# Multiplying a 64-row weight tail as two half-array products

## The reference

```
w    = softmax(weight, axis=-1)                 # 8 heads, 7 taps
conv[s, head] = sum_k w[head, k] * x[s + k - 6, head]      # causal, along the sequence
h1   = conv @ w_in1      (192 x 2048);  g1 = h1 * cos(h1);               y1 = g1 @ w_out1
h2   = y1 @ w_in2        (192 x 2048);  g2 = h2 * clip(h2 + 3, 0, 6)/6;  out = g2 @ w_out2
```

## Time and profile before

| | us |
|---|---|
| median of 3 runs | 2409.83 (2409.76 to 2409.97) |
| the profiled execution | 2408.54 |
| its span, first to last instruction | 2406.8 |
| TensorE matmul busy | 2367.1 (98%) |
| VectorE busy | 1776.7 (74%) |
| ScalarE busy | 1495.7 (62%) |
| GpSimd busy | 1313.7 (55%) |

### The profile page before, as it was taken

How to read it: one execution, slowest core, us unless ns; L and a number is a source line. 1 busy time by engine, 2 the same in 40 slices (tenths; PEclk the granted TensorE clock), 3 DMA queues, 4 the chain that set the end, 5 groups by cost and what they waited for, 6 DMA issues and landing times.

```text
span 2406.8 us, 32826 instructions
## 1 busy us (share of the span) xinstructions
PE 2367.1 (98%) x10254; PEld 1929.2 (80%) x10254; DVE 1776.7 (74%) x2253; ACT 1495.7 (62%) x1748; POOL 1313.7 (55%) x543
## 2 busy tenths in 40 slices
PE   5999999999999999999999999999999999999998
PEld 3788888888888888888888888888888888888886
DVE  8777776777767777767777677777677776777753
ACT  4765566665666655666656666566666566665663
POOL 6755555555555555555555555555555555555554
PEclk8999999999999999999999999999999999999999
DMA  4100000000000000000000000000000000000001
GB/s 110 38 1 13 7 7 13 13 13 13 0 13 13 13 13 7 7 13 13 13 13 0 13 13 13 13 6 7 13 13 13 13 0 13 13 13 13 3 4 20
DMA packets 208226, 32.76 MB, mean 14 GB/s; under 512 B 203088, under 2 KB 207184, under 8 KB 208208
## 3 DMA queue, kind: packets, MB, share of 16 engines
q1 hardware_dynamic: 208208, 32.53, 7.7%
HBM read 19.92 MB, written 12.58 MB: 14 GB/s over the span
## 4 chain that ended last, share of the span: by engine, by line
PE 97%; DVE 1%; issue 1%; DMA 1%; SPq 0%; ACT 0%; POOL 0%; DVEq 0%; POOLq 0%; ACTq 0%
PE h_ps L347 10%; PE h_ps L346 10%; PE acc L366 10%; PE acc_tail L368 10%; PE h_ps L349 10%; PE acc L365 10%; PE acc_tail L369 10%; PE h_ps L348 10%; PE h_ps L350 10%; PE acc L367 10%; DMA gate<-in_moe_w_out 1%; DVE pre L520 0%; DVE gate L533 0%; DVE in_ftail L580 0%; DVE in_f L580 0%
## 5 line engine op out<-in xcount | busy, mean ns | idle before, releaser
L690 POOL TENSOR_TENSOR g_lo<-gate,g_hi 128x1024 fp32r<-128x1024 f32 x512 | 1270.2, 2481 | 1070.0 <-ACT g_hi L442 1069.7
L428 ACT ACTIVATE pre<-h_ps,three 128x1024 f32<-128x1024 f32 x256 | 286.7, 1120 | 547.0 <-PE h_ps L350 547.0
L442 ACT ACTIVATE g_hi<-gate 128x1024 fp32r<-128x1024 f32 x512 | 538.8, 1052 | 31.7 <-DVE gate L533 31.2
L520 DVE TENSOR_TENSOR pre<-pre,h_ps 128x1024 f32<-128x1024 int32 x256 | 311.9, 1218 | 257.3 <-ACT pre L426 257.3
L535 DVE SCALAR_TENSOR_TENSOR gate<-pre,h_ps 128x512 f32<-128x512 f32 x512 | 327.3, 678 | 214.5 <-ACT pre L428 213.5
L533 DVE TENSOR_TENSOR gate<-pre,h_ps 128x512 f32<-128x512 f32 x512 | 331.6, 685 | 129.4 <-ACT pre L436 126.0
L346 PE MATMUL h_ps<-in_hi,win_hi 128*128 128x512 f32 x1024 | 406.1, 397 | 18.7 <-DVE gate L533 9.9
L426 ACT ACTIVATE pre<-h_ps 128x1024 int32<-128x1024 f32 x256 | 262.4, 1025 | 232.5 <-PE h_ps L350 232.5
L347 PE MATMUL h_ps<-in_lo,win_hi 128*128 128x512 f32 x1024 | 406.1, 397 | 0.0
L349 PE MATMUL h_ps<-in_tail,wtail_hi 128*128 128x512 f32 x1024 | 403.4, 394 | 0.0
L366 PE MATMUL acc<-g_lo,wout 128*128 128x512 f32 x1024 | 402.6, 393 | 0.0
(11 more groups left out here) (69 smaller groups left out, 2225.8 us busy)
## 6 DMA issues: line engine op xcount, KB each, us to landing
x_in<-in_x SPq DMA_DIRECT2D x128, 64.0 KB, 2.2
out_dram<-o_blk SPq DMA_DIRECT2D x128, 64.0 KB, 1.8
blk_tail<-in_x SPq DMA_DIRECT2D x64, 64.0 KB, 2.2
out_dram<-blk_tail SPq DMA_DIRECT2D x64, 64.0 KB, 1.8
stage<-in_moe_w_out SPq DMA_DIRECT2D x6, 384.0 KB, 3.2
stage<-in_moe_w_in SPq DMA_DIRECT2D x3, 512.0 KB, 3.7
stage<-in_moe_w_in SPq DMA_DIRECT2D x6, 256.0 KB, 4.1
gate<-in_moe_w_out SPq DMA_DIRECT2D x2, 384.0 KB, 12.2
```

Of the source, the lines that this page charges most:

```text
L442: act.activation(g_hi[:, q % G_BUFS, :], gate[:, q % 2, :], ACT.Copy).then_inc(ghi_ready, 1)
L690: pool.tensor_tensor(g_lo[:, n, :], gate[:, q % 2, :], g_hi[:, n, :].bitcast(F32), ALU.subtract).then_inc(glo_ready, 1)
```

## The change

The low part of w_in's tail is kept once instead of twice, and packed: of a slot's two chunks, the even one lies in rows 0 to 63 of `wtail_lo`, the odd one in rows 64 to 127, in the same 128 columns. The two L350 matmuls of 128 rows are replaced by two of 64 rows that stand together after the slot's other eight: chunk 0 by rows 0 to 63 of `in_tail` (the tail's high part), chunk 1 by rows 64 to 127 of `in_twin`, a new tile into which ScalarE copies the same high part. The product of the low weights with the low input of the tail is no longer made. TensorE waits on a new signal, `twin_ready`. GpSimd splits such a weight block with two subtractions, one for each half of the rows, and waits in between for work of its own.

```diff
-        wtail_lo = [sb(f"wtail_lo{n}", [P, FF], F32R) for n in (1, 2)]
+        wtail_lo = [sb(f"wtail_lo{n}", [P, FF // 2], F32R) for n in (1, 2)]
+        in_twin = [sb(f"in_twin{n}", [P, TOK], F32R) for n in (1, 2)]
...
+        def every_other(a, rows, odd):
+            return a[rows, :].rearrange("p (c t f) -> p c t f", t=2, f=P)[:, :, odd, :]
...
-                hi = (win_hi if i % 2 == 0 else wtail_hi)[layer][:, cols]
-                lo = (win_lo if i % 2 == 0 else wtail_lo)[layer][:, cols]
                 src = buf[:, 0:HALF_FF]
-                return (src, hi), [(src, hi, lo)]
+                if i % 2 == 0:
+                    hi = win_hi[layer][:, cols]
+                    return (src, hi), [(src, hi, win_lo[layer][:, cols])]
+                hi = wtail_hi[layer][:, cols]
+                lo = wtail_lo[layer][:, (i // 2) * HALF_FF // 2:(i // 2 + 1) * HALF_FF // 2]
+                return (src, hi), [(every_other(src, rows, odd), every_other(hi, rows, odd),
+                                    lo[rows, :].rearrange("p (c f) -> p c f", f=P))
+                                   for odd, rows in enumerate((slice(0, DT), slice(DT, P)))]
...
-                    last = pe.matmul(dst, wtail_lo[layer][:, c], in_tail[source][:, :], start=False, stop=True)
+                for half, rows, tail in ((0, slice(0, DT), in_tail), (1, slice(DT, P), in_twin)):
+                    c = slice(q * P, (q + 1) * P)
+                    last = pe.matmul(chunk_of(h_ps, q, half), wtail_lo[layer][rows, c], tail[source][rows, :],
+                                     start=False, stop=True)
                 last.then_inc(h_ready, 1)
...
                         pe.wait_ge(lo_ready[ph.source], 2 * (ph.tile + 1 + (ph.source != ph.layer)))
+                        pe.wait_ge(twin_ready[ph.source], ph.tile + 1 + (ph.source != ph.layer))
...
                         pe.wait_ge(lo_ready[L1], 4)
+                        pe.wait_ge(twin_ready[L1], 2)
...
                 act.activation(in_hi[to][:, :], in_f[layer][:, :], ACT.Copy).then_inc(hi_ready[to], 1)
+                act.activation(in_twin[to][DT:P, :], in_ftail[layer][:, :], ACT.Copy).then_inc(twin_ready[to], 1)
                 act.activation(in_tail[to][0:DT, :], in_ftail[layer][:, :], ACT.Copy).then_inc(hi_ready[to], 1)
...
-            def weight_low(b):
+            def weight_low(b, slots_done):
                 pool.wait_ge(whi_done, b + 1)
-                for src, hi, lo in parts_of(b)[1]:
-                    last = pool.tensor_tensor(lo, src, hi.bitcast(F32), ALU.subtract)
-                last.then_inc(wlo_done, 1)
+                parts = parts_of(b)[1]
+                if b % BLOCKS not in (1, 3):
+                    for src, hi, lo in parts:
+                        last = pool.tensor_tensor(lo, src, hi.bitcast(F32), ALU.subtract)
+                    last.then_inc(wlo_done, 1)
+                    return
+                pool.wait_ge(wlo_done, b)
+                if slots_done > 0:
+                    pool.wait_ge(glo_ready, slots_done)
+                (src, hi, lo), (src2, hi2, lo2) = parts
+                pool.tensor_tensor(lo, src, hi.bitcast(F32), ALU.subtract).then_inc(tail_split, 1)
+                pool.wait_ge(tail_split, 2 * (b // BLOCKS) + b % BLOCKS // 2 + 1)
+                pool.tensor_tensor(lo2, src2, hi2.bitcast(F32), ALU.subtract).then_inc(wlo_done, 1)
+                pool.wait_ge(wlo_done, b + 1)
```

More of the change, by code:

```diff
@@ L171, in conv_moe_kernel @@
         lo_ready = [sem(f"lo{n}_ready") for n in (1, 2)]
+        twin_ready = [sem(f"twin{n}_ready") for n in (1, 2)]
         o_turned = sem("o_turned")
@@ L178, in conv_moe_kernel @@
         wlo_done = sem("wlo_done")
+        tail_split = sem("tail_split")
         w_loaded = sem("w_loaded")
@@ L707, in _ @@
             for b in range(BLOCKS):
-                weight_low(b)
+                weight_low(b, 0)
             for slot in range(2 * SLOTS):
@@ L712, in _ @@
                 if block_now is not None:
-                    weight_low(block_now)
+                    weight_low(block_now, slot)
                 low_part(slot, slot, slot >= G_BUFS)
```

## The result

The changed kernel takes 2497.44 us (2497.24 to 2497.66) against 2409.82: ratio 1.0363, 95% interval 1.0347 to 1.0378. It is 87.6 us slower. The direction was forecast, the size was not: 202 us were predicted, and the price per slot comes out at 0.17 us instead of 0.40.

A forecast was written before the change was run, and what follows sets the result against it. TensorE's matmul count times spacing was taken as the bound; +0.40 us per slot over 505 slots gave 202 us on a 2406.8 us span, so 2612 us median. Its own range was 2506 to 2690, stretched down to 2345.

The forecast's parts named there:

- the sum per slot: Two changes of shape 0.52 us, plus 0.11 second load, minus 0.23 saved spacing: net +0.40 us per slot.
- the emptying: TensorE drains before loading weights, into and out of the pair: 0.15 us each, between 0.10 and 0.20.
- the open load inside the pair: The second 64-row matmul's weight load can only follow the first's: +0.11 us per slot.
- TensorE's spacing is the time, and all other edits cost nothing: Nearly everywhere time is matmul count times 0.229 us spacing; ScalarE's extra copy, waits and GpSimd's split add nothing.
- The saving of one spacing by overlap: The two 64-row matmuls run at once in separate row halves: −0.23 us per slot.
- A change of shape empties the array and then opens the weight load, twice per slot: Into the pair and out of it, 0.15 us emptying plus 0.11 us open load each: 0.52 us per slot.
- the tap products: L335 (8x128) and L336 (8x64), which spread the taps; L336's load read as 0.20 us late at half clock.
- the recorded tail of a matmul: A steady-stream matmul record lasts 0.39 us at 0.23 us spacing, leaving 0.16 us; used to choose the emptying's size.
- rival A: Nothing empties and both 64-row matmuls overlap: faster, 2305 us, or 2349 with the second load open; chance 0.20.
- lower bound of +0.19: Least net cost per slot: 0.10 us emptying and 0.11 us load twice, second load hidden, one spacing saved.
- B: No overlap and no emptying, 20 spacings remain: 2410 us; chance 0.08, together with gain and cost cancelling.
- C: Emptying, but loads stay hidden: +0.07 to +0.18 us per slot, 2445 to 2501 us; chance 0.06.

The follow-up runs named there:

- full_rows: Changed kernel with the 64-row pair replaced by two 128-row products at the same place, all other edits kept: 2410.59 us.
- same_rows: Changed kernel with both 64-row products of a slot in rows 0 to 63 of the array: 2621.98 us.
- one_half: Changed kernel with each slot's second 64-row product (the odd chunk's, rows 64 to 127) left out: 2487.31 us.
- pair_apart: Changed kernel with the two 64-row products apart, each behind its own chunk's four products, so four changes of shape per slot: 2817.50 us.
- triple_pair: Changed kernel with the 64-row pair issued three times over in each slot, without further changes of shape: 2723.58 us.
- pairs_spread: Against the kernel before: all main-loop products as 64-row pairs, 19 per slot, with VectorE's and ScalarE's side work spread over more slots: 2377.65 us.
- pairs_late_low: pairs_spread with in_lo subtracted whole before the fraction, and each phase begun with the two pairs that need only in_hi: 2373.65 us.

## Why the prediction was wrong

The mechanism was right, and two terms of the sum per slot were too large: the emptying, taken at 0.15 us and measured at 0.09, twice per slot, and the open load inside the pair, taken at 0.11 us and measured at nothing.

- *TensorE's spacing is the time, and all other edits cost nothing.* Right: full_rows is equal within 0.1%. The spacing itself was read a little short: the 437 of the earlier trace rows counts every matmul that touches the window, and 435 begin in it, so it is 0.230 us and the slot 4.60, not 4.58. That changes nothing in the difference. The phases hand over without a stall, and ScalarE's busy time rose by 46 us for nothing (40 forecast).
- *The saving of one spacing by overlap.* Right: same_rows costs 0.244 us more, one_half saves only 0.020.
- *A change of shape empties the array and then opens the weight load, twice per slot.* Right: the loads come late by the chain of distances above, and pair_apart pays 0.20 us for each further change. The rule of the Trainium skill ("TensorEngine Tiling (Array Packing)", section Tiling Modes) that a change of mode drains TensorE holds here, and the price is 0.09 us at full clock and 0.13 at half clock, besides the open load.
- *"I take 0.15 us" for the emptying.* This is the term that was mis-sized most: it measures 0.09 us, twice per slot, 0.12 us too much. I had read 0.20 us at half clock from the tap products and then let the recorded tail of a matmul decide. At half clock this change shows 0.13 us, so the tap products (which change columns, have 7 columns and a second pass) are no measure for this one; and at full clock the time is shorter, two thirds of it. The recorded tail is no measure, since its end is modelled and the load does not wait for it: the load begins 0.07 us ahead of it (1002.41 + 0.39 against 1002.73), as in the earlier trace rows, which I had seen and not used.
- *"+0.11" for the second load, which "can only follow the first's".* Wrong: both halves load at the same time (1002.73 and 1002.73). The Trainium skill ("TensorE: Matmul & The Clock Gate", Part 3) has products on different row groups start about 4 ns apart; the trace agrees within its 0.01 us. It stood in rival A, and I charged the load in the forecast all the same. 0.11 us too much.
- The sum with the measured terms: 2 x (0.09 + 0.11) − 0.23 = +0.17, by the row of each phase 0.172. My lower bound of +0.19 had hidden the second load and put 0.10 for the emptying, so that form of the case was the right one, and 0.02 too high. The measured 2497 us lie just below the forecast's own lower bound of 2506 for that reason. Of the 0.40 forecast, 0.12 and 0.11 were the excess of the two terms.
- *Rivals.* A fails, its gain of 0.23 is there but is outweighed by 0.40 of changes. B fails. C fails, the loads are open; that the measured time lies within its 2445 to 2501 us is luck, since it left out the open loads and took the emptying too large.

Not settled: why the ordinary distances of the second product are a few nanoseconds shorter in one_half and triple_pair than in the changed kernel. They carry the 0.020 us that one_half saves, and the 0.02 us by which triple_pair's slot grew less than its pairs' stretch.

## What to carry to other kernels

A pair of half-height products in the two halves of the array does run in the time of one, loads included, but entering and leaving that shape costs about 0.2 us each way at full clock, nearly a 512-column product each. By these numbers a visit pays only if it saves at least two spacings (0.46 us against 0.40, an estimate; triple_pair points the same way, since its slot of 5.22 us does the work of 24 full products at 0.23, 5.52 us). What the runs show is that it pays if the loop never leaves the shape, full products cut into halves too. When the first engine gets faster, look for the side work that stands between a value and the gate that needs it: moving such pieces, and letting TensorE begin a phase with the pairs whose input comes first, was worth 142 us here. The first of these moves, tried alone in the kernel before, was worth nothing.

## What the runs showed of the hardware

- The emptying at a change of rows in use takes 0.09 us at clock 1.00 and 0.13 us at clock 0.50: neither a fixed time nor a fixed number of array cycles by these two.
- A product of 128 rows cut into two halves for different banks runs in 0.232 us where the whole takes 0.230: 38 products and 38 loads in 4.40 us are no bound for TensorE's queue.
- A VectorE subtraction of two SBUF operands that begins while GpSimd's subtraction runs seems to do its work only behind it: with 512 columns it ends 0.54 to 0.56 us after GpSimd's (all 65 such in the kernel before, whenever they began), with 256 columns 0.28 to 0.30 (pairs_spread). So 0.69 us became 2.76 (L678), and 256 columns of in_lo took 0.45 or 2.62. In_lo's 2.39 us in the earlier trace rows are the same wait: GpSimd's subtraction beside it ends at 1027.67, in_lo at 1028.22. In pairs_late_low it begins 0.17 us before GpSimd's end and takes 0.72 us. In the kernel before, TensorE covers the wait. The other way round VectorE is not held up: in_tail's subtraction takes its 0.68 us when GpSimd's begins while it runs.

```profile
1025.27 2.40 POOL L690 TENSOR_TENSOR g_lo<-gate,g_hi 128x1024 fp32r<-128x1024 f32 x1 [1.78 <-ACT g_hi L442]
```
